# Piece sizes of q and k in the first stage, and the place of ScalarE's two table loads in tile 4

## The chip, the cores and the metric

The kernel runs on one core of a Trainium2 chip. The time is the device time of one execution in microseconds; where several runs are given, it is their median. TensorE multiplies, ScalarE and VectorE work elementwise and move results out of PSUM, GpSimd (POOL) and SyncE (SP) mostly issue DMAs. Each engine works through its own instructions in order and waits on semaphores.

## The reference

Two batches of an attention over channels, whose output goes token by token through a two-layer network:

```python
def _attn_ref(q, k, v, tau):            # each (2, 6016, 256), float32
    qn = q / (np.linalg.norm(q, axis=1, keepdims=True) + 1e-06)
    kn = k / (np.linalg.norm(k, axis=1, keepdims=True) + 1e-06)
    s = kn.transpose(0, 2, 1) @ qn / tau        # 256 x 256 a batch
    s = s - s.max(-1, keepdims=True)
    a = np.exp(s)
    a /= a.sum(-1, keepdims=True) + 1e-09
    return (v @ a).astype(np.float32)

def _moe_ref(x, w_in, w_out, alpha):    # x (12032, 256), w_in (256, 2048), w_out (2048, 256)
    h = x @ w_in
    g = np.maximum(h, 0.0) + alpha * np.minimum(h, 0.0)
    return (g @ w_out).astype(np.float32)
```

## The kernel before

The kernel has two parts. The first, up to about 57 us, reads q and k of batch 0 in 47 blocks of 128 tokens (a block is 128 x 512 numbers, q and k side by side, 256 KB) and makes the scores k^T q with TensorE, a block at a time, into one PSUM bank (`qk_block`, L444). Each of its products is two matmul instructions of float32, so a block is four. The blocks arrive in pieces: `PIECES = [2, 3] + [4] * 10 + [2]` (L51) gives the blocks of each piece, and each piece is one DMA on SP's queue into one of `RING = 7` buffers called `stage` (L279). SP issues the first seven at once; for each later one it waits until TensorE and ScalarE are done with the piece that had the buffer. Behind them on SP's queue stand w_in, v of the first tile and nine `late` blocks of batch 1.

Beside it the norms are made, which need the sums of the squares over the tokens. `SUBS` (L59) cuts every piece in parts of at most two blocks. For each part ScalarE squares it (L775) and VectorE adds the squares to `acc0` (L1053); behind the last, VectorE folds two blocks to one (L1056). TensorE then sums over the partitions with a matrix of ones (`channel_sums`, L473). In TensorE's order the sums stand behind the third piece from the end, that is with two pieces still to go (L570). From the sums go: VectorE's clamp (L934), ScalarE's root (L683) with the load of the exponential's table behind it (L686), VectorE's inverse norms and a diagonal matrix (L941 to L952), TensorE's broadcast of the norms of q (`broadcast_rq`, L479) when all 47 blocks are done, ScalarE's copy of that row (L690), VectorE's scaling of the scores (L960), the exponentials (L695) and TensorE's transposes (`transpose_probs`, L486), which stand behind four late blocks in TensorE's order. In VectorE's order splits and sums of v (L894, L903 to L912) are written between the steps of this chain. Ahead of everything TensorE multiplies zeros (`keep_warm`, L440) and opens the two banks of scores with zeros (L435).

The attention matrix is multiplied into w_in, which gives the matrix M of the network's first layer; products with M are made by a scheme of seven multiplications for a 2 x 2 block product. All operands are split into a high and a low part, and each product is three matmuls (hi hi, hi lo, lo hi).

The second part is the main loop: 12 tiles of up to 1024 tokens, each with 8 groups, G = 0 to 95. A group makes in TensorE's order (L597 to L640) the products in the banks Y, X and Z, then three more into X, each followed or preceded by the second layer's products of the group before (`down`, L538). It takes 45 products of 512 columns. ScalarE copies X out four times a group (`take_x`, L747), once behind each product in X; TensorE's next product in X waits for the copy. Between the copies ScalarE casts the high parts of g (L757) and of v (L659) and, in chosen groups, does other work: in tile 4 (groups 32 to 39) the norms, the root, the exponentials and the transposes of batch 1. Group 33 is `SUMS_G`, in which VectorE makes the sums of the squares; group 34 is `ROOT_G`, in which ScalarE takes the root behind its first copy of X; 35 is `BROADCAST_G`. ScalarE needs a table load ahead of the root and another ahead of the exponentials. Both are brought about by a one-column activation: at the end of group 33 the square root (L859), at the end of group 34 the exponential (L686, `load_exp`).

Of the kernel before, what the change touches and what calls it, by code (L numbers as in the profile page):

```python
# [5 lines left out]
def build(nc, qk, qk_t, v_t, w_in, w_out, small, y_t):  # L6
# [4 lines left out]
    ACT = mybir.ActivationFunctionType  # L11
# [20 lines left out]
    def half_width(T):  # L32
        t = T % TILES
        return HALF if t < TILES - 1 else (N - 2 * HALF * (TILES - 1)) // 2
# [13 lines left out]
    SLOT = {B11: 0, T1: 0, T2: 0, T3: 1, B21: 2, T4: 2, B22: 3}  # L48


    PIECES = [2, 3] + [4] * 10 + [2]  # L51
    assert sum(PIECES) == NBLK
    START = [sum(PIECES[:i]) for i in range(len(PIECES))]
    RING = 7
# [3 lines left out]
    assert LATE + 2 * PAIRS == NBLK  # L58
    SUBS = [(i, n, min(2, PIECES[i] - n)) for i in range(len(PIECES)) for n in range(0, PIECES[i], 2)]  # L59
    PAIR_TILES = (1, 2, 3)  # L60
# [18 lines left out]
    with ctx:  # L79
        def sb(name, shape, dt=fp32):  # L80
            return ctx.enter_context(nc.sbuf_tensor(name, shape, dt))
# [8 lines left out]
        ones = sb("ones", [P, P])  # L90
# [7 lines left out]
        warm = sb("warm", [P, 1])  # L98
# [156 lines left out]
        SUMS_G, ROOT_G, BROADCAST_G, SCALE_G, EXP_G, MOVE_G = (SOFT + n for n in range(6))  # L255
# [14 lines left out]
        def side(k):  # L270
            return sigma_neg if BLOCKS[k][1] else sigma
# [4 lines left out]
        def _(sp):  # L276
            def load_piece(i):
                n0, n1 = START[i], START[i] + PIECES[i]
                sp.dma_start(stage[:, i % RING, 0:PIECES[i], :].rearrange("p n c -> p (n c)"),  # L279
                             qk[0, :, n0 * ROW:n1 * ROW]).then_inc(stage_loaded[i % RING], 16)  # L280
# [57 lines left out]
            sp.dma_start(small_sb[:, :], small[:, :]).then_inc(small_loaded, 16)  # L338
            for i in range(RING, len(PIECES)):
                sp.wait_ge(qk0_summed, i - RING + 1)  # L340
# [305 lines left out]
        def _(act):  # L646
# [34 lines left out]
            def take_root(b):  # L681
                act.wait_ge(sumsq_ready, b + 1)
                nc.scalar.activation(root, sum_sq, ACT.Sqrt).then_inc(root_ready, 1)  # L683

            def load_exp():
                nc.scalar.activation(warm[:, :], ones[:, 0:1], ACT.Exp)  # L686

            def copy_rq(b):
                act.wait_ge(rq_bc_ready, b + 1)
                nc.scalar.copy(rq_row, bc_ps).then_inc(rq_row_ready, 1)  # L690

            def exponentials(b):
                act.wait_ge(max_ready, b + 1)
                for kc in range(CC):
                    nc.scalar.activation(probs[:, kc, :], scores[:, kc, :], ACT.Exp,  # L695
                                         bias=neg_max[:, kc:kc + 1],
                                         accum_out=row_sum[:, kc:kc + 1]).then_inc(exp_ready, 1)
# [39 lines left out]
            def take_x(G, n, k):  # L737
                T, jp = G // JP, G % JP
                H = half_width(T)
                j = 2 * jp + BLOCKS[k][0]  # L740
                act.wait_ge(x_done, 4 * G + n + 1)
                if G > 0:
                    act.wait_ge(g_lo_ready, 4 * (G - 1) + k + 1)
                else:

                    act.wait_ge(sums_ready, 1)
                nc.scalar.mul(h[:, k, 0:H], X[:, 0:H], side(k)[:, j:j + 1]).then_inc(x_copied, 1)  # L747

            def split_g_hi(G, k):
                H = half_width(G // JP)  # L750
                act.wait_ge(g_ready, 4 * G + k + 1)
                if G > 0:
                    act.wait_ge(down_done, 4 * (G - 1) + k + 1)
                else:

                    act.wait_ge(m_done, M_FIRST)
                nc.scalar.copy(g_hi[:, k, 0:H], h[:, k, 0:H]).then_inc(g_hi_ready, 1)  # L757

            def take_y(T, t, oc):
                H = half_width(T)  # L760
                act.wait_ge(down_done, 4 * (JP * T + JP - 1) + 3 + t)
                if T == 0:

                    act.wait_ge(w_lo_ready, FJ)
                else:
                    act.wait_ge(y_stored[t], 16 * T)
                nc.scalar.copy(y_stage[:, t, oc, 0:H], y_ps[t][oc][:, 0:H]).then_inc(y_copied, 1)
# [39 lines left out]
            for G in range(GROUPS):  # L807
                T, jp = G // JP, G % JP
                take_x(G, 0, 0)
                if jp == 1 and T > 0:  # L810
                    take_y(T - 1, 1, 0)
                if G > 0:
                    split_g_hi(G - 1, 3)
                if jp == 1 and T > 0:
                    take_y(T - 1, 1, 1)
                if G == ROOT_G:
                    take_root(1)
                if G == EXP_G:
                    exponentials(1)
                if G == 0:  # L820
                    split_m_hi(0, 1)
                if G == 2:
                    split_m_hi(0, 3)
                if G in M_SPLIT:
                    split_m_hi(*M_SPLIT[G])
                if T + 1 < ALL:
                    for op in (V_ACT_FIRST if T == 0 else V_ACT).get(jp, ()):
                        if T == 0 and op == B11:

                            act.wait_ge(qk1_summed, len(LATE_STEPS))  # L830
                        split_v_hi(T + 1, op)
                take_x(G, 1, 3)
                if G == 0:
                    take_m(0, 2)
                if G in PAIR_AT:
                    split_pair_hi(PAIR_AT[G])
                if G == BROADCAST_G:
                    copy_rq(1)
                if G == MOVE_G:
                    split_at_hi(1)  # L840
                if G in M_AT:
                    take_m(*M_AT[G])
                take_x(G, 2, 1)
                split_g_hi(G, 0)
                if G == 0:
                    split_m_hi(0, 2)
                for n in SQ_AT.get(G, ())[:1]:
                    square_rows(n)
                take_x(G, 3, 2)
                if G == 0:  # L850
                    take_m(0, 3)
                for k in (1, 2) if G < GROUPS - 1 else (2, 1):
                    split_g_hi(G, k)
                if jp == 0 and T > 0:
                    take_y(T - 1, 0, 0)
                for n in SQ_AT.get(G, ())[1:]:
                    square_rows(n)
                if G == SUMS_G:
                    nc.scalar.activation(warm[:, :], ones[:, 0:1], ACT.Sqrt)  # L859
                if G == ROOT_G:  # L860
                    load_exp()
                if G in SLICE_AT:
                    split_slice_hi(SLICE_AT[G])
                for j in W_AT.get(G, ()):
                    split_w_hi(j)
# [331 lines left out]
```

## Time and profile before

| | |
|---|---|
| median of 3 runs | 1076.53 us (1076.34 to 1077.75) |
| the profiled execution, its own time | 1076.63 us |
| its span, first to last instruction | 1074.8 us |
| TensorE matmul, busy | 1070.9 us, 100% |
| TensorE weight load, busy | 906.2 us, 84% |
| VectorE, busy | 847.0 us, 79% |
| ScalarE, busy | 654.6 us, 61% |
| GpSimd, busy | 40.4 us, 4% |

A matmul is counted as busy from its start to its modelled end, and they overlap, so that 100% says that TensorE always has something in hand, not that it never waits. Waits show as idle time of its weight loads (PEld) and as matmuls that take longer than their like. Times in rows are in us from the start of the span; "[0.37 <-ACT ...]" is the idle time of the engine ahead of the instruction, and who ended it.

### The profile page before, as it was taken

The page shows a single profiled execution, that of the slowest core. Times are in us where ns is not written, and L with a number is a line of the kernel's source. Part 1 is how long each engine was busy: PE and PEld are TensorE (multiplying, and loading weights), DVE is VectorE, ACT ScalarE, POOL GpSimd, SP SyncE. Part 2 cuts the span into 40 slices and gives each one's busy share as a digit, 9 for nine tenths or more (in the row PEclk, how much of TensorE's full clock was granted, in tenths as well). Part 3 has the DMA queues.
Part 4 walks back from the last instruction along what each step waited for, and adds up shares of the span by engine and source line. Part 5 has one row for each costly group of instructions (what it writes and reads, how often), then busy time and mean ns, then how long its engine had stood idle before and what let it go on. Part 6 is the DMA issues. An engine that isn't in the chain of part 4 may idle for free.

```text
span 1074.8 us, 13902 instructions
## 1 busy us (share of the span) xinstructions
PE 1070.9 (100%) x4995; PEld 906.2 (84%) x4995; DVE 847.0 (79%) x1349; ACT 654.6 (61%) x1100; POOL 40.4 (4%) x54
## 2 busy tenths in 40 slices
PE   9999999999999999999999999999999999999998
PEld 7888888888888888888998888888888888888898
DVE  6999987877877777787798887777777777787776
ACT  6676677667766555655666655555555555555544
POOL 0000000000000000000000000000000000000000
PEclk9999999999999999999999999999999999999999
DMA  9621154455453102103212101201202202200101
GB/s 382 284 88 50 40 158 127 138 160 150 134 162 99 30 13 54 45 9 79 69 30 73 50 11 49 59 8 52 59 1 59 59 0 54 57 1 10 40 1 35
DMA packets 30837, 80.07 MB, mean 74 GB/s; under 512 B 2992, under 2 KB 9264, under 8 KB 29232
## 3 DMA queue, kind: packets, MB, share of 16 engines
q1 hardware_dynamic: 24288, 67.80, 18.1%
q0 software_dynamic: 6336, 11.28, 6.8%
q8 instruction: 39, 0.64, 0.2%
q14 instruction: 30, 0.25, 0.1%
q10 hardware_dynamic: 144, 0.11, 0.0%
HBM read 64.04 MB, written 12.32 MB: 71 GB/s over the span
## 4 chain that ended last, share of the span: by engine, by line
PE 100%; ACT 0%; issue 0%; POOL 0%; POOLq 0%
PE y_ps L538 47%; PE x_ps L512 24%; PE z_ps L512 12%; PE p_ps L512 6%; PE x_ps L444 4%; PE s_ps L464 3%; PE p_ps L498 2%; PE s_ps L444 1%; PE y_ps L498 1%; PE y_ps L553 0%; PE z_ps L440 0%; PE p_ps L486 0%; PE p_ps L473 0%; PE p_ps L479 0%; ACT y_stage L876 0%; PE s_ps L435 0%
## 5 line engine op out<-in xcount | busy, mean ns | idle before, releaser
L538 PE MATMUL y_ps<-g_hi,w_hi 128*128 128x512 f32 (+1 forms) x760 | 293.1, 386 | 0.0
L538 PE MATMUL y_ps<-g_hi,w_lo 128*128 128x512 f32 (+1 forms) x760 | 292.9, 385 | 0.0
L538 PE MATMUL y_ps<-g_lo,w_hi 128*128 128x512 f32 (+1 forms) x760 | 292.9, 385 | 0.0
L757 ACT CAST g_hi<-h 128x512 fp32r<-128x512 f32 (+1 forms) x384 | 234.0, 610 | 78.6 <-DVE h L1011 69.3
L1011 DVE SCALAR_TENSOR_TENSOR h<-h,small_sb 128x512 f32<-128x512 f32 (+1 forms) x384 | 273.7, 733 | 0.0
L1003 DVE SCALAR_TENSOR_TENSOR h<-z_ps,sigma_neg,h 128x512 f32<-128x512 f32 (+1 forms) x192 | 141.7, 738 | 148.0 <-ACT h L747 147.6
L1045 DVE TENSOR_TENSOR g_lo<-h,g_hi 128x512 fp32r<-128x512 f32 (+1 forms) x384 | 249.9, 670 | 0.8 <-ACT g_hi L757 0.5
L747 ACT ACTIVATE h<-x_ps,sigma_neg 128x512 f32<-128x512 f32 (+1 forms) x192 | 130.7, 681 | 175.2 <-PE x_ps L512 165.1
L747 ACT ACTIVATE h<-x_ps,sigma 128x512 f32<-128x512 f32 (+1 forms) x192 | 130.6, 680 | 124.8 <-PE x_ps L512 120.2
L538 PEld LDWEIGHTS y_ps<-g_hi,w_hi 128*128 128x128 f32 x760 | 142.7, 188 | 27.3 <-issue 0.3
L538 PEld LDWEIGHTS y_ps<-g_hi,w_lo 128*128 128x128 f32 x760 | 142.7, 188 | 27.0
L538 PEld LDWEIGHTS y_ps<-g_lo,w_hi 128*128 128x128 f32 x760 | 142.7, 188 | 26.6
L512 PE MATMUL x_ps<-v_hi,m_hi 128*128 128x512 f32 (+1 forms) x384 | 148.8, 388 | 0.0
L512 PE MATMUL x_ps<-v_lo,m_hi 128*128 128x512 f32 (+1 forms) x384 | 148.1, 386 | 0.0
L512 PE MATMUL x_ps<-v_hi,m_lo 128*128 128x512 f32 (+1 forms) x384 | 148.0, 385 | 0.0
L1003 DVE SCALAR_TENSOR_TENSOR h<-p_ps,sigma,h 128x512 f32<-128x512 f32 (+1 forms) x96 | 70.8, 738 | 42.2 <-ACT h L747 42.2
L512 PEld LDWEIGHTS x_ps<-v_hi,m_hi 128*128 128x128 f32 x384 | 72.1, 188 | 14.4 <-ACT h L747 0.9
L512 PEld LDWEIGHTS x_ps<-v_hi,m_lo 128*128 128x128 f32 x384 | 72.1, 188 | 13.6
L512 PEld LDWEIGHTS x_ps<-v_lo,m_hi 128*128 128x128 f32 x384 | 72.1, 188 | 12.9
L512 PE MATMUL z_ps<-v_hi,m_hi 128*128 128x512 f32 (+1 forms) x192 | 74.3, 387 | 0.0
L512 PE MATMUL z_ps<-v_lo,m_hi 128*128 128x512 f32 (+1 forms) x192 | 74.0, 385 | 0.0
L512 PE MATMUL z_ps<-v_hi,m_lo 128*128 128x512 f32 (+1 forms) x192 | 73.9, 385 | 0.0
(129 smaller groups left out, 1009.4 us busy)
## 6 DMA issues: line engine op xcount, KB each, us to landing
rows_t<-qk_t SPq DMA_DIRECT2D x32, 376.0 KB, 4.0
stage<-qk SPq DMA_DIRECT2D x10, 1024.0 KB, 13.3
v_stage<-v_t SPq DMA_DIRECT2D x20, 512.0 KB, 4.6
y_t<-y_stage SPq DMA_DIRECT2D x20, 512.0 KB, 2.8
pair<-qk SPq DMA_DIRECT2D x19, 512.0 KB, 3.7
v_stage<-v_t POOLq DMA_DIRECT2D x27, 256.0 KB, 4.1
scratch<-w_in SPq DMA_DIRECT2D x12, 256.0 KB, 2.8
v_stage<-v_stage POOLq DMA_DIRECT2D x9, 256.0 KB, 3.3
```

The costliest lines, as they stand in the source:

```text
L444: product = nc.tensor.matmul(s_ps[b][:, kc * C:(kc + 1) * C], rows[:, C + kc * P:C + (kc + 1) * P], rows[:, 0:C], start=False, stop=last, ...
L464: product = nc.tensor.matmul(S[:, kc * C:(kc + 1) * C], k_part[:, i, ks], q_part[:, i, 0:C], start=False, stop=n == PAIRS - 1 and i == 1 a ...
L498: product = nc.tensor.matmul(bank[:, kc * 2 * P:(kc + 1) * 2 * P], a_part[:, qc, kc * P:(kc + 1) * P], w_part[:, qc, :], start=a_part is a ...
L512: product = nc.tensor.matmul(bank[:, 0:H], m_part[:, jp, a, :], v_part[T % 2][:, t, 0:H], start=start and m_part is m_hi and v_part is v_h ...
L538: product = nc.tensor.matmul(y_ps[t][oc][:, 0:H], w_part[:, j, ws], g_part[:, k, 0:H], start=jp == 0 and k < 2 and w_part is w_hi and g_pa ...
L747: nc.scalar.mul(h[:, k, 0:H], X[:, 0:H], side(k)[:, j:j + 1]).then_inc(x_copied, 1)
L757: nc.scalar.copy(g_hi[:, k, 0:H], h[:, k, 0:H]).then_inc(g_hi_ready, 1)
L1003: return nc.vector.scalar_tensor_tensor(out=h[:, k, 0:H], in0=bank[:, 0:H], scalar=side(k)[:, j:j + 1], in1=h[:, k, 0:H], op0=ALU.mult, op ...
L1011: nc.vector.scalar_tensor_tensor(out=h[:, k, 0:H], in0=h[:, k, 0:H], scalar=alpha_sb[:, j:j + 1], in1=h[:, k, 0:H], op0=ALU.mult, op1=ALU. ...
L1045: nc.vector.tensor_tensor(g_lo[:, k, 0:H], h[:, k, 0:H], g_hi[:, k, 0:H].bitcast(fp32), ALU.subtract).then_inc(g_lo_ready, 1)
```

## The change

`PIECES` goes from 2, 3, ten of 4 and 2 to 1, 2, 3, ten of 4 and 1: 14 pieces in place of 13, over the same 47 blocks and the same ring of seven buffers. The loops over the pieces, the parts of at most two blocks (25 in place of 24) and all waits follow from this list. The two activations that bring in the tables in groups 33 and 34 move, in ScalarE's order, from the end of the group to a place behind the second copy of X.

```diff
@@ -48,7 +48,7 @@
-    PIECES = [2, 3] + [4] * 10 + [2]
+    PIECES = [1, 2, 3] + [4] * 10 + [1]
     assert sum(PIECES) == NBLK
@@ -830,6 +830,10 @@
                 take_x(G, 1, 3)
+                if G == SUMS_G:
+                    nc.scalar.activation(warm[:, :], ones[:, 0:1], ACT.Sqrt)
+                if G == ROOT_G:
+                    load_exp()
                 if G == 0:
                     take_m(0, 2)
@@ -855,10 +859,6 @@
                 for n in SQ_AT.get(G, ())[1:]:
                     square_rows(n)
-                if G == SUMS_G:
-                    nc.scalar.activation(warm[:, :], ones[:, 0:1], ACT.Sqrt)
-                if G == ROOT_G:
-                    load_exp()
                 if G in SLICE_AT:
```

## Rows read from the trace of the kernel before

**Rows 1.** The page, chain of work that ended last, shares by engine.
```profile
PE 100%; ACT 0%; issue 0%; POOL 0%; POOLq 0%
```
**Rows 2.** Waits of TensorE's weight loads, 30 us to the end: total, times, longest.
```profile
PEld x_ps L512 <- ACT h L747: 0.9, 3, 0.4
...
PEld p_ps L486 <- ACT scratch L695: 0.4, 1, 0.4
```
**Rows 3.** DMA issues, 0 to 10 us (KB, us to landing); timeline (start, us): first products.
```profile
stage<-qk SPq DMA_DIRECT2D x1, 512.0 KB, 3.8
...
4.62 36.37 PE L444 MATMUL x_ps<-stage 128*128 128x256 f32 x164
```
**Rows 4.** Timeline of TensorE's matmuls in narrow windows, 3 to 10 us.
```profile
3.54 0.63 PE L435 MATMUL x_ps<-zeros 128*128 128x512 bf16 x1
3.96 0.63 PE L435 MATMUL s_ps<-zeros 128*128 128x512 bf16 x1
...
7.81 1.46 PE L444 MATMUL x_ps<-stage 128*128 128x256 f32 x6
```
**Rows 5.** Timeline, 5 to 42 us: SP's reloads, VectorE's sums, fold, low parts.
```profile
7.36 16.73 SPq L279 DMA_DIRECT2D stage<-qk  x6
...
26.20 11.86 DVE L1053 TENSOR_TENSOR acc<-acc,sq 128x1024 f32<-128x1024 f32 x9 [0.28 <-ACT sq L775]
...
38.10 0.69 DVE L1056 TENSOR_TENSOR acc<-acc 128x512 f32<-128x512 f32 x1
...
39.40 2.50 DVE L1024 TENSOR_TENSOR w_raw_lo<-w_raw,w_raw_hi 128x512 fp32r<-128x512 f32 x4
```
**Rows 6.** Timeline, 40 to 51 us: from the channel sums to the transposes.
```profile
40.83 1.05 PE L473 MATMUL p_ps<-ones,acc 128*128 128x128 f32 x8
...
41.92 0.16 DVE L934 TENSOR_SCALAR col<-p_ps 128x4 f32<-128x4 f32 x1
...
46.91 0.59 PE L479 MATMUL p_ps<-scratch,ones 128*128 128x256 f32 x2
46.92 0.69 DVE L909 TENSOR_TENSOR v_stage<-v_stage 128x512 f32<-128x512 f32 x1
...
47.94 0.88 DVE L960 SCALAR_TENSOR_TENSOR scratch<-x_ps,col,scratch 128x256 f32<-128x256 f32 x2 [0.33 <-ACT scratch L690]
...
50.92 0.42 PEld L486 LDWEIGHTS p_ps<-ident,scratch 128*128 128x128 f32 x4 [0.37 <-ACT scratch L695]
```
**Rows 7.** Chain that ended last in order of time, 428 to 470 us.
```profile
438.90 0.68 PE z_ps L512 x3
...
440.94 0.74 PE x_ps L512 x3
...
443.07 0.84 PE x_ps L512 x3
443.91 1.39 PE y_ps L538 x6
```
**Rows 8.** Timeline, 428 to 450 us: ScalarE's copies of X, table loads, VectorE, TensorE.
```profile
428.74 0.69 ACT L747 ACTIVATE h<-x_ps,sigma 128x512 f32<-128x512 f32 x1 [0.17 <-PE x_ps L512]
...
433.50 0.69 ACT L747 ACTIVATE h<-x_ps,sigma_neg 128x512 f32<-128x512 f32 x1 [1.35 <-PE x_ps L512]
...
434.29 0.75 DVE L1003 SCALAR_TENSOR_TENSOR h<-z_ps,sigma_neg,h 128x512 f32<-128x512 f32 x1 [1.94 <-ACT h L747]
...
434.66 0.39 PE L512 MATMUL x_ps<-v_hi,m_hi 128*128 128x512 f32 x1
...
438.58 1.28 ACT L859 ACT_TABLE_LOAD   x1
...
439.99 0.67 ACT L747 ACTIVATE h<-x_ps,sigma 128x512 f32<-128x512 f32 x1
...
442.20 0.69 ACT L747 ACTIVATE h<-x_ps,sigma_neg 128x512 f32<-128x512 f32 x1 [0.48 <-DVE g_lo L1045]
...
448.79 1.28 ACT L686 ACT_TABLE_LOAD   x1
```

## The prediction

> **What bounds the kernel now.** I read the chain of waits on the page first: it ends last through TensorE at 100% of the span [rows 1]. The reader should see there that nothing off TensorE can shorten the kernel; only a stall of TensorE, or work of its own, is worth anything. But this chain also counts a stretched matmul as work, so the second view is the list of what its weight loads waited for, from 30 us on [rows 2]. It holds two small things that touch this diff: three waits on ScalarE's copies of X, 0.9 us together, and one wait of 0.4 us for the exponentials ahead of the transposes. Everything that the change can move lies in three places: the first 7 us, the chain from the channel sums to the transposes (41 to 51 us), and groups 33 and 34 at 428 to 450 us. I take them in that order.
>
> **The start: a first piece of one block.** TensorE's warm-up ends with two matmuls of 512 columns, the openings of the score banks, which start at 3.54 and 3.96 [rows 4]; 512 columns in 0.42 us is the lower of the engine's two levels, 1.2 GHz. (The granted clock of the windows prints 1.00 there too, so I go by the spacing.) The first product of q and k starts at 4.62 [rows 3], as soon as the first piece of two blocks, 512 KB, has landed: 0.74 + 3.8 = 4.54 [rows 3]. One block less is about 0.62 us less of transfer, an estimate from 256 KB at the 426 GB/s that this stretch moves; so it lands near 3.9 and is no longer the limit. The limit is then the opening at 3.96 plus 0.42 = 4.38. TensorE starts 0.24 us earlier.
>
> What is that worth? At the upper level a product's matmuls are 0.216 us apart ((1.46 - 0.38) / 5, [rows 4]). All 164 at that pace would be 163 x 0.216 + 0.38 = 35.6 us; the row says 36.37 [rows 3], so 0.78 us was lost at the start, that is 0.37 on a first step of 0.59 and 0.21 on each of two of 0.43. The clock therefore rose near 4.62 + 0.59 + 2 x 0.43 = 6.07. If it rises at the same time again, TensorE fits between 4.38 and 6.07 about one matmul more: it is ahead by g = 0.2 us from there on. The bounds: 0.14 if the long first step stays, 0.24 if all of it counts; zero if the small piece lands no earlier, since the first packets are slow ones. I take 0.2.
>
> Does TensorE then starve? The pieces stand at 1, 3, 6, 10 and 14 blocks; at 0.62 us each behind 3.9 they land near 5.2, 7.1, 9.6 and 12.1. TensorE (0.864 us a block, four matmuls of 0.216) wants them at 6.1, 7.8, 10.4 and 13.9. No starvation, by 0.6 us at the least. ScalarE squares one more piece and VectorE adds it: the count of instructions goes from 24 to 25, and three of them are of one block instead of one. A sum of two blocks comes every 1.33 us ((11.86 - 1.23) / 8, [rows 5]); for one of one block I estimate 0.8 from half the elements: 22 x 1.33 + 3 x 0.8 against 23 x 1.33 + 0.8 is 0.3 us more. The last fold starts at 38.10 [rows 5] and TensorE comes to the channel sums only at 40.83 [rows 6]; 2 us of cover hide it. VectorE's work behind the fold, the low parts of w_in, ends at 41.90 [rows 5], and would end by 42.2. SP's queue: the reloads of the ring wait for smaller early pieces, but they lie so far ahead of the transfers (issued from 7.36 to 24.1, [rows 5]) that the DMA engines keep a backlog; w_in, v and the late blocks, queued behind, move by 0.1 to 0.4 us at most, and TensorE wants the late blocks only at 47.
>
> **The sums one block later.** This is the part that costs. TensorE takes the channel sums at the third piece from the end. Before, 41 blocks stand ahead of them (2 + 3 + 9 x 4) and 6 behind; now 42 and 5. So the sums start 0.86 - g = 0.66 us later, near 41.49 by [rows 6]. What waits for them: VectorE's clamp at 41.92, which starts just as the sums end, and behind it in VectorE's queue everything up to the end of the mixing at 46.92 + 0.69 = 47.61, a stretch without a gap worth naming; behind ScalarE's root its table load and its copies, which have 3 us to spare. VectorE then stood idle for ScalarE's copy of the norms' row and started the scaling of the scores at 47.94 [rows 6]: 0.33 us, of which 0.04 is handshake. That is all the slack of this chain, 0.3. TensorE's own order (47 blocks, sums, broadcast at 46.91) does not change; it only comes 0.2 earlier. So the scaling starts at max(47.65 + 0.66, 47.94 - 0.2) = 48.3, 0.36 later than before; reduction, exponentials and transposes follow one another without another path, and TensorE's wait ahead of the transposes, 0.37 us at 50.92 [rows 6], starts 0.2 earlier and ends 0.36 later: near 0.93 us. Afterwards every engine stands behind this same point, so the delay is kept. Head: **+0.36 us**, between +0.6 (g = 0, no slack) and -0.2 (the chain has slack I do not see, and g is kept).
>
> **The table loads in tile 4.** The square root's load stands at the end of group 33, ahead of the first copy of X of group 34. It takes 1.28 us at 438.58, and that copy starts at 439.99 [rows 8], where the groups' period of 10.20 (45 matmuls of 0.2267) and the same copy of group 33 [rows 8] put it at 428.74 + 10.20 = 438.94. The delay passes through VectorE's sum and low part to the second copy, at 442.20 instead of 441.66 (431.46 + 10.20, and 431.46 is 433.50 - 1.35 - 0.69), and so into TensorE: in the chain in order of time four pieces of this group are stretched, 0.74, 1.39 (twice) and 0.84, where three matmuls take 0.68 and six 1.36 [rows 7]. That is 0.06 + 0.03 + 0.16 + 0.03 = 0.28 us. The exponential's load at 448.79 [rows 8] stretches nothing: the next group is longer only by its broadcast.
>
> Behind the second copy, ScalarE is idle for 1.35 us before the third, waiting for TensorE [rows 8]. Load and warm-up take 439.99 - 438.58 = 1.41. The third copy is thus late by some 0.06 to 0.1 us in both groups. What is queued behind: that copy, then the casts of g and the fourth copy. TensorE wants the third at 434.66 and it ends at 433.50 + 0.69 = 434.19 [rows 8]; 0.47 us of cover against 0.1. VectorE's add of Z behind it, 434.29 + 0.75, is wanted by the product in Z at 434.66 + 0.68 = 435.34: 0.3 of cover. So the new place costs nothing and the 0.28 comes back. Bounds: 0.15 if the root and the cast keep the second copy late, 0.28 if not. Tile 4: **-0.28 us**.
>
> A rule that speaks against this half: the Trainium skill (ScalarE: Activation LUTs, What ACT_TABLE_LOAD costs) gives each switch 1.28 us for the load and 1.38 for a drain, 2.66 together. The trace agrees on the first and not on the second: the load starts 0.02 behind the end of the cast before it, and the copy follows at once. By the rule the answer would be the last rival below.
>
> **Sum.** 1076.63 us is the profiled execution's own time, its span 1074.8 and 1.8 around it; + 0.36 - 0.28 gives 1076.7. It lies 0.1 above the median of the three runs, so I say **1076.6** for a median. The three runs spread over 1.4 us, more than both terms.
>
> **The rivals.** (a) Forecast, both terms as above: 1076.6, chance 0.50. (b) The first piece brings nothing (its packets are no quicker than the landing seen), and the second copy in group 34 stays half late: + 0.57 - 0.15, 1076.95, slower than before; decided by whether the first product still starts at 4.6. Chance 0.20. (c) The chain behind the sums has more slack than the 0.3, for instance if VectorE's small steps are quicker when nothing else runs: head - 0.2, total - 0.48, 1076.05. Against it speaks the stretch without gaps. Chance 0.12. (d) The clock rises earlier, because TensorE no longer pauses between 4.38 and 4.62; nothing in the trace dates it but the one rise. At most the whole stretch to 6.07 at the upper level: g near 1.0, since each of the four or so slow steps then gives 0.21 more; the sums come earlier than before and everything moves with them: - 0.4 - 0.28, 1075.85. Chance 0.08. The Trainium skill (TensorE: Matmul & The Clock Gate, Part 1) says that the place of the rise varies from run to run; no row here shows that. (e) ScalarE is held for 2.66 us by each load in its new place, from 432.15 to 434.8: the third copy ends 0.95 us after TensorE wants it, in both groups, and the switch decides as soon as it takes over 1.8 us. + 1.9 + 0.36 - 0.28: 1078.5. Chance 0.03. The rest, 0.07, is for what I have not seen, on both sides.
>
> **Range and chances.** 1075.8 to 1077.5 takes in (a) to (d) with their bounds and the spread of a median of three; it leaves out (e) and half the rest. A measurement can tell about 0.2%, 2.15 us, from no change; only (e) and the unseen come near: faster by more than that 0.02, slower 0.03, the same 0.95.
>
> **What would show it.** Right: the first product near 4.4; eight matmuls of the sums near 41.5 and the clamp near 42.6; VectorE no longer idle ahead of the scaling, which starts near 48.3; the wait ahead of the transposes near 0.9 us; the stretched pieces at 441 to 444 back to 0.68 and 1.36; the third copies of groups 33 and 34 less than 0.15 later in their group. Wrong: TensorE waiting for a piece or for the fold, an idle VectorE ahead of the clamp with no later end, a stretched piece around 434 or 445.

## The result and the profile after

The changed kernel takes 1078.28 us in the median of 22 runs (1077.44 to 1079.58), the kernel before, on the same chips, 1077.09 (22 runs, 1076.34 to 1078.03). The ratio is 1.0013, 95% interval 1.0007 to 1.0019: about 1.2 to 1.4 us slower. The forecast was 1076.6, in a range of 1075.8 to 1077.5; it started from a median of 1076.53 for the kernel before, so 0.5 of the 1.7 us between forecast and measurement is that starting value, and the change itself was forecast at about + 0.1 and measured at + 1.2. The profiled execution took 1079.16 us, its span is 1077.3; it lies 0.9 above the median of its kernel, so not all that it shows need belong to the typical run.

The chain of work that ended last is no longer TensorE alone. From the page after:

```profile
PE 98%; DVE 1%; DMA 1%; ACT 0%; issue 0%; SPq 0%; DVEq 0%; ACTq 0%
```

Where [rows 1] had TensorE at 100%, there is now a DMA, and VectorE. The waits of TensorE's weight loads, 5 to 30 us (total, times, longest), where the kernel before has none:

```profile
PEld x_ps L444 <- DMA stage<-qk: 1.4, 1, 1.4
```

The first transfers after (count, KB, us to landing):

```profile
stage<-qk SPq DMA_DIRECT2D x1, 768.0 KB, 7.0
stage<-qk SPq DMA_DIRECT2D x1, 512.0 KB, 3.8
stage<-qk SPq DMA_DIRECT2D x1, 256.0 KB, 2.8
```

The start of the timeline after (start, us, what):

```profile
3.58 0.63 ACT L775 ACTIVATE sq<-stage 128x512 f32<-128x512 f32 x1 [0.48 <-DMA stage<-qk]
...
4.06 1.52 SPq L338 DMA_DIRECT2D small_sb<-small  x1
...
4.39 3.35 PE L444 MATMUL x_ps<-stage 128*128 128x256 f32 x12
...
8.69 1.13 PE L444 MATMUL x_ps<-stage 128*128 128x256 f32 x4 [0.95 <-DMA stage<-qk]
```

The first product starts at 4.39, against 4.62 in [rows 3]: as forecast. But behind three blocks (twelve matmuls) TensorE stands still from 7.7 to 8.7, until the third piece lands; the forecast had it at 7.1. ScalarE waits for the same piece, and VectorE behind it. A stretch by stretch view of both kernels shows why (window, then busy us of five engines with their counts; last three: granted clock, DMA share, GB/s). Before, then after:

```profile
4.00:5.00 1.00, 0.97 (x3) 0.38 (x2) 0.00 (x0) 0.40 (x1) 0.00 (x0) 1.00 1.05 440
5.00:6.00 1.00, 1.00 (x3) 0.80 (x3) 0.23 (x1) 0.66 (x1) 0.00 (x0) 1.00 1.01 424
6.00:7.00 1.00, 1.00 (x6) 0.83 (x5) 0.99 (x1) 0.51 (x1) 0.00 (x0) 1.00 1.06 451
7.00:8.00 1.00, 1.00 (x6) 0.90 (x5) 0.42 (x1) 1.00 (x2) 0.00 (x0) 1.00 0.99 418
```
```profile
4.00:5.00 1.00, 1.00 (x4) 0.82 (x3) 0.68 (x1) 0.22 (x2) 0.00 (x0) 1.00 1.01 385
5.00:6.00 1.00, 1.00 (x5) 0.83 (x4) 0.01 (x1) 1.00 (x1) 0.00 (x0) 1.00 0.88 352
6.00:7.00 1.00, 1.00 (x7) 0.87 (x6) 0.92 (x1) 0.04 (x1) 0.00 (x0) 1.00 1.09 371
7.00:8.00 1.00, 0.73 (x4) 0.30 (x2) 0.30 (x1) 0.00 (x0) 0.00 (x0) 1.00 0.96 344
```

The DMA engines are nearly as busy as before (shares of 0.88 to 1.09 against 0.99 to 1.06) and move 344 to 385 GB/s in place of 418 to 451. By the packets in the traces, nine of the 311 that start between 3 and 8 us take two to five times as long as is usual for their size; before, none of 333 does.

The other places. The channel sums and what follows (after, beside [rows 6]):

```profile
43.55 0.16 DVE L934 TENSOR_SCALAR col<-p_ps 128x4 f32<-128x4 f32 x1 [0.20 <-PE p_ps L473]
...
49.17 0.87 DVE L960 SCALAR_TENSOR_TENSOR scratch<-x_ps,col,scratch 128x256 f32<-128x256 f32 x2
...
52.14 0.42 PEld L486 LDWEIGHTS p_ps<-ident,scratch 128*128 128x128 f32 x4 [0.82 <-ACT scratch L695]
```

VectorE is no longer idle ahead of the scaling, and the wait ahead of the transposes is 0.82 us where it was 0.37. Tile 4, the chain in order of time after (beside [rows 7]):

```profile
442.21 0.68 PE x_ps L512 x3
442.89 1.36 PE y_ps L538 x6
444.25 0.68 PE x_ps L512 x3
```

And the timeline of ScalarE in group 33 after (beside [rows 8]):

```profile
433.41 1.28 ACT L834 ACT_TABLE_LOAD   x1
434.70 0.20 ACT L834 ACTIVATE warm<-ones 128x1 f32<-128x1 f32 x1
434.81 0.67 ACT L747 ACTIVATE h<-x_ps,sigma_neg 128x512 f32<-128x512 f32 x1
```

The stretched pieces are back at 0.68 and 1.36: group 34 takes 10.22 us in place of 10.48. And one place that the forecast did not look at, in tile 5 (batch 1's first M, 549 us). The chain in order of time after:

```profile
547.80 0.35 issue
...
549.18 0.02 DVEq L1128
549.20 0.40 issue
549.60 0.70 DVE h L1003
550.29 0.04 issue
550.34 0.86 PE z_ps L512 x3
```

Before, at the same work, the chain is TensorE without a break:

```profile
548.35 0.62 PE x_ps L512 x3
548.97 0.63 PE z_ps L512 x3
```

Between VectorE's wait, which is over at 549.20, and its add of Z at 549.60 nothing happens for 0.40 us, "issue" in the page's words; before, the same add started 0.05 behind its wait. The product in Z waits for this add. From one fourth copy of X to the next, group 45 takes 11.02 us in place of 10.63.

So the profiled execution reads: + 1.22 us up to the end of group 0 (67.55 against 66.32, the fourth copy of X), - 0.26 in group 34, + 0.39 in group 45, + 0.12 in group 44, and + 0.67 in the last four groups, whose matmuls are 0.2066 apart in place of 0.2027. This last term comes and goes: near the end of the span, e1 has it in four groups, e9 and e10 in three, e13 in two, e2, e8 and e15 in one, most of the others in none. I count it as a matter of the single execution; that is a judgement, not shown.

### The profile page after: what moved, and what is told of

The parts are those of the page before. It is cut to its first block, busy times and chain, and to the rows that moved or that the text cites. A ratio compares the mean times of both kernels' runs of the same rounds, so it can differ in the third digit from the quotient of the medians.

```text
span 1077.3 us, 13908 instructions
## 1 busy us (share of the span) xinstructions
PE 1071.9 (99%) x4995; PEld 906.7 (84%) x4995; DVE 847.2 (79%) x1350; ACT 655.2 (61%) x1101; POOL 40.5 (4%) x54
## 4 chain that ended last, share of the span: by engine, by line
PE 98%; DVE 1%; DMA 1%; ACT 0%; issue 0%; SPq 0%; DVEq 0%; ACTq 0%
PE y_ps L538 47%; PE x_ps L512 24%; PE z_ps L512 12%; PE p_ps L512 6%; PE x_ps L444 3%; PE s_ps L464 3%; PE p_ps L498 2%; DMA stage<-qk 1%; PE y_ps L498 1%; PE y_ps L553 0%; PE s_ps L444 0%; DVE v_lo L894 0%; ACT scratch L695 0%; PE p_ps L486 0%; PE p_ps L473 0%
## 5 line engine op out<-in xcount | busy, mean ns | idle before, releaser
L1003 DVE SCALAR_TENSOR_TENSOR h<-p_ps,sigma,h 128x512 f32<-128x512 f32 (+1 forms) x96 | 70.8, 738 | 41.5 <-ACT h L747 41.4
```

What stands on the lines that cost most here:

```text
L1003: return nc.vector.scalar_tensor_tensor(out=h[:, k, 0:H], in0=bank[:, 0:H], scalar=side(k)[:, j:j + 1], in1=h[:, k, 0:H], op0=ALU.mult, op ...
```

## The experiments

Three questions: does each half cost what was forecast; why does the third piece land late; where does VectorE's pause come from. The table has one row for each kernel, from its own profile: first product, VectorE's clamp, fourth copy of X of group 0 (all us from the start of the span), length of groups 34 and 45, and its ratio to the kernel before where it ran six times or more, or else the time of its one run (the kernel before, on the same chips, took 1076.85 beside e5 and e6, 1077.06 beside e11 and 1077.20, one run, beside e13 to e16).

| kernel | first product | clamp | group 0 | group 34 | group 45 | ratio (95%) |
|---|---|---|---|---|---|---|
| before | 4.62 | 41.92 | 66.32 | 10.48 | 10.63 | |
| after | 4.39 | 43.55 | 67.55 | 10.22 | 11.02 | 1.0013 (1.0007 to 1.0019) |
| e1 pieces 1, 2, 3 ... 1 alone | 4.39 | 43.18 | 67.17 | 10.47 | 11.02 | 1.0012 (1.0003 to 1.0021) |
| e2 loads alone | 4.88 | 41.88 | 66.03 | 10.23 | 10.75 | 0.9997 (0.9988 to 1.0006) |
| e3 pieces 1, 1, 3 ... 2 | 4.39 | 44.78 | 68.78 | 10.49 | 11.02 | 1.0031 (1.0020 to 1.0043) |
| e4 pieces 2, 4 ... 1 | 4.62 | 42.83 | 66.84 | 10.49 | 10.63 | 1.0006 (0.9997 to 1.0015) |
| e5 first piece in two DMAs | 4.40 | 44.44 | 68.59 | 10.47 | 10.63 | one run, 1078.84 us |
| e6 first piece in two halves of rows | 5.56 | 43.76 | 67.74 | 10.47 | 10.63 | one run, 1077.99 us |
| e7 pieces 1, 4 ... 2 | 4.39 | 42.03 | 66.44 | 10.46 | 10.68 | 1.0002 (0.9993 to 1.0011) |
| e8 VectorE shifted | 4.72 | 41.73 | 65.86 | 10.46 | 10.68 | 1.0006 (0.9997 to 1.0015) |
| e9 VectorE shifted, two waits | 4.57 | 41.68 | 66.07 | 10.46 | 10.68 | 1.0005 (0.9996 to 1.0014) |
| e10 after, burst of six | 4.39 | 42.87 | 66.85 | 10.22 | 10.99 | 1.0009 (1.0000 to 1.0018) |
| e11 long burst of issues | 4.43 | 50.04 | 74.01 | 10.47 | 10.75 | one run, 1084.50 us |
| e12 loads, early broadcast | 4.64 | 42.28 | 66.27 | 10.23 | 10.72 | 0.9996 (0.9987 to 1.0005) |
| e13 pieces 4, 1, 1 ... 1 | 5.83 | 44.88 | 68.89 | 10.47 | 10.99 | one run, 1079.86 us |
| e14 pieces 1, 3 ... 3 | 4.39 | 42.33 | 66.32 | 10.47 | 10.99 | one run, 1076.97 us |
| e15 pieces 2, 2, 3 | 4.75 | 41.94 | 66.38 | 10.47 | 10.63 | one run, 1076.88 us |
| e16 third piece held | 4.39 | 42.94 | 66.92 | 10.47 | 10.99 | one run, 1077.80 us |

A warning on the first three columns. TensorE's clock rises at another moment in each profile (6.09 in before, 5.58 in after, 4.55 in e1 and e2, 3.65 to 6.67 in all but e13, by the granted clock and by the spacing of the matmuls, 0.427 us ahead of the rise and 0.216 behind it), and a rise that comes 1 us earlier gives back about 0.5 us. So differences of some tenths in group 0 between two profiles are read with the place of the rise beside them.

### The halves and the two terms of the sum

e1 takes the new list without the moved loads, e2 the moved loads without the new list.

> The new piece list alone, the table loads where they were before. Theory A (the third piece of q and k lands late whenever the first pieces are this small: TensorE waits 1.1 us for it at 8.5 us, as in the profile of after, and the sums come one block later): 1.2 to 1.5 us slower than the kernel before, with a wait of TensorE for a piece near 7.4 us in the trace. Theory B (that wait was a chance of the one profiled execution; only the later sums cost): 0.3 to 0.5 us slower, no such wait.

> The moved table loads alone, pieces as before. If the change of place gives back the stretched matmuls of group 34 and nothing else moves: 0.25 us faster than before, group 34 at 10.20 to 10.23 us in place of 10.48. Rival (it disturbs something later, as the longer groups 44 and 45 in the profile of after): 0 to 0.6 us slower.

e1 is as slow as both together, and TensorE waits for the third piece again (its weight loads 1.0 us, in after 1.4): theory A. But the wait is not the whole of its price. In e1 the clock rose 1.5 us earlier than before, so that TensorE had made up for the wait when it came to block 41; still the clamp is 1.26 us later than before, and it starts 0.55 us behind the sums' end, because VectorE is not done (timelines of VectorE and TensorE in e1):

```profile
40.77 2.50 DVE L1024 TENSOR_TENSOR w_raw_lo<-w_raw,w_raw_hi 128x512 fp32r<-128x512 f32 x4
41.58 1.05 PE L473 MATMUL p_ps<-ones,acc 128*128 128x128 f32 x8
43.18 0.16 DVE L934 TENSOR_SCALAR col<-p_ps 128x4 f32<-128x4 f32 x1
```

The low parts of w_in start 1.37 us later than in [rows 5]. VectorE's own chain of sums stands behind the late piece too and has one part more. In after TensorE ends this wait (sums to 43.51, low parts to 43.35), in e3, e5, e6, e10 and e16 VectorE does, as in e1.

e2 shows the forecast gain in its place, 10.23 us for group 34, but its time is not told from that of the kernel before: the 0.25 us is less than its 11 runs can tell.

```diff
e3: -    PIECES = [2, 3] + [4] * 10 + [2]
    +    PIECES = [1, 1, 3] + [4] * 10 + [2]
e4: +    PIECES = [2, 4] + [4] * 10 + [1]
e7: +    PIECES = [1, 4] + [4] * 10 + [2]
```

> Pieces 1, 1, 3, ten of 4 and 2: the first piece small, the sums at the same block as before (41 ahead, 6 behind), loads as before. Theory A (small first pieces make a later piece land late): 0.5 to 1.2 us slower, with a wait of TensorE for a piece before 10 us. Theory B (a small first piece lets TensorE start 0.24 us earlier and costs nothing): 0.15 to 0.2 us faster, first product near 4.3.

> Pieces 2, 4, ten of 4 and 1: the first piece as before, the sums one block later (42 ahead, 5 behind), loads as before. By the prediction's sum for g = 0: 0.5 to 0.6 us slower, the wait ahead of the transposes near 0.9 us in place of 0.37, the scaling idle-free. Rival (the chain has slack): no slower than 0.1.

> Pieces 1, 4, ten of 4 and 2: a small first piece, then large ones; sums at the same block, as many parts as before (24). Theory D: packets slow at 3 to 7 us, piece 4 lands after 8.5 us, over 1 us slower than before. Theory C or none: TensorE waits some 0.4 us for the second piece (five blocks at 6.4), 0.2 us slower than before at most.

e4 isolates the later sums: from its waits,

```profile
PEld p_ps L486 <- ACT scratch L695: 0.8, 1, 0.8
```

with group 0 ending 0.52 us later and 0.65 us in time (not clear of zero by its interval). The forecast's sum for g = 0 was 0.57. This term was right in place and about right in size: two smaller things nearly cancel in e4's profile, a short wait for its larger second piece (two steps of 0.41 and 0.32 us in place of 0.22) and a clock that rose 0.5 us earlier. e3 keeps the sums where they were and is the slowest of those timed more than once: 3.3 us by the ratio. (Four of its six runs, 1080.6 to 1081.2 us, have a mean granted clock of 0.998; the two at 1.0 took 1078.9 and 1079.7, so 2.1 to 3.0 us of it stand without that.) e7, with the same small first piece but a large second one, is at most 1.2 us slower by its interval and has only a short wait for its second piece:

```profile
PEld x_ps L444 <- DMA stage<-qk: 0.5, 1, 0.5
```

So a small first piece alone does not bring the long wait. What the earlier start is worth, e7 does not show: its first product is 0.23 us earlier, but its sixth matmul starts at 6.62 in place of 6.52, since its clock rose at 6.51 in place of 6.09 (0.2 us) and it waited 0.1 us for the second piece. Three profiles with the first pieces of the kernel before do show what a lead is worth. Their clock rose earlier, their sums start earlier than the 40.83 of [rows 6], and group 0 ends earlier by the same amount: e2 0.31 and 0.29 us, e8 0.46 and 0.46, e9 0.26 and 0.25.

### Why the third piece is late

```diff
 e5, first piece of the kernel before in two DMAs, both awaited:
+                if i == 0:
+                    for part in range(2):
+                        sp.dma_start(stage[:, 0, part, :], qk[0, :, part * ROW:(part + 1) * ROW]
+                                     ).then_inc(stage_loaded[0], 16)
+                    return
 ...
 e6, the same, but 64 partitions and both blocks in each:
+                        ps = slice(part * P // 2, (part + 1) * P // 2)
 ...
```

> The kernel before, but its first piece of two blocks comes as two DMAs of one block each, and TensorE and ScalarE wait for both as for one. Theory D (small rows at the head of the queue make the DMA engines themselves slow, whoever uses the data): packets behind them slow between 3 and 7 us, below 180 KB in each half microsecond in place of 210, a wait of TensorE for the third piece near 7 us, as in the kernel with pieces 1, 1, 3. Theory C (the engines that start early on the small piece disturb the transfers): transfers and first waits as in the kernel before.

> The kernel before, but its first piece comes as two DMAs of 64 partitions each, rows of 4 KB as before. If it is the size of the rows (2 KB against 4 KB) that makes the engines slow: as the kernel before. If it is one more DMA in the queue, or a DMA of half the bytes: slow as the split by blocks.

e5 does what the kernel before does, only its first 512 KB come as two DMAs, and they land 0.2 us sooner. It moves 313 to 379 GB/s from 4 to 8 us (windows of e5), and TensorE waits 3 us for the next piece (waits of e5):

```profile
4.00:5.00 1.00, 1.00 (x4) 0.51 (x3) 0.00 (x0) 0.62 (x1) 0.00 (x0) 1.00 0.81 313
...
7.00:8.00 1.00, 0.00 (x0) 0.00 (x0) 0.00 (x0) 0.00 (x0) 0.00 (x0) 1.00 0.99 358
```
```profile
PEld x_ps L449 <- DMA stage<-qk: 3.7, 2, 3.0
```

Already from 3 to 4 us, when no engine uses q and k yet, it moves 344 GB/s against 426 before. The engines that use the data are thus not the cause. e6 is slow too, though not as long (166, 350, 391 and 410 GB/s; its waits for pieces: 2.7 us), with rows of 4 KB as before: the size of the rows is not needed for it. Its halves of 64 partitions may do something of their own, so it carries less weight.

The next two ask whether it is SP's issuing beside the transfers (its eighth issue took 1.52 us after, 0.45 before).

```diff
 e10, on the changed kernel:
             for i in range(RING):
+                if i == 6:
+                    sp.wait_ge(stage_loaded[2], 16)
                 load_piece(i)
 e11, on the kernel before:
             sp.dma_start(small_sb[:, :], small[:, :]).then_inc(small_loaded, 16)
+            for part in range(len(LATE_PARTS)):
+                load_late(part)
+            load_v(0)
 ... (and their calls further down go)
```

> The changed kernel, but SP issues six pieces at once and holds the seventh and what is behind it until the third has landed; the DMA engines keep work until 14 us. Theory B (the transfers are slow when the third DMA of the queue moves while SP still issues its first ones): now SP is done at 3.4 us, ahead of the third piece at 3.9; packets at full pace, third piece lands near 7.1, no wait of TensorE for it, first part 1.1 us shorter than in the changed kernel, time 0.2 to 0.5 us above the kernel before. Rival (small DMAs are slow by themselves): slow as the changed kernel, 1.2 us above the kernel before.

> The pieces of the kernel before, but v of the first tile and the late blocks are issued right behind the small constants, so that SP issues twelve DMAs without a wait, until about 6.5 us. Theory B: the third piece starts to move at 5.4 us, while SP still issues: packets slow from then on, issues of 1 us and more, third piece of four blocks lands after 9.6 in place of 9.0. Rival: packets at full pace to the end. The total time says nothing here, since the late blocks now stand ahead of the eighth piece and TensorE waits for it later.

Both went against theory B. In e10 SP is silent from 3.6 us until the third piece has landed, and the transfers are slow all the same (330, 332, 352, 367 GB/s in the four windows from 4 to 8 us); its time, 0.85 us above the kernel before by the medians, lies between the two expectations. In e11 SP issues without a pause to 6.9 us, and they run at full pace:

```profile
5.00:6.00 1.00, 1.00 (x6) 0.87 (x5) 0.42 (x1) 0.47 (x1) 0.00 (x0) 1.00 1.06 442
```

(e11's time of 1084.5 us says nothing of this: its weight loads wait 4.5 us for a later piece, and behind that wait the granted clock is at the lower level, 0.50, from 29.0 to 35.8 us.) The long issue is a companion of the slowness, not its cause. The last four vary the sizes and the time alone.

```diff
e13: +    PIECES = [4, 1, 1] + [4] * 10 + [1]
e14: +    PIECES = [1, 3] + [4] * 10 + [3]
e15: +    PIECES = [2, 2, 3] + [4] * 10
e16: the new list, and
             for i in range(RING):
+                if i == 2:
+                    sp.wait_ge(stage_loaded[0], 16)
                 load_piece(i)
```

> Pieces 4, 1, 1, ten of 4 and 1. Theory E (slow when the third DMA of the queue starts to move within some 3 us of the first packet): here the third starts near 5.0 us; packets at full pace, about 210 KB in each half microsecond from 3 us on. Theory S (two DMAs of at most two blocks one behind the other): slow, 160 to 180 KB in each half microsecond from 5 us on. The time says little, TensorE starts 1.2 us later.

> Pieces 1, 3, ten of 4 and 3: one small DMA, then one of three blocks; the third starts near 4.8 us. Theory S: full pace, as pieces 1, 4. Theory E: at its border, full pace or a little slow. Sums one block earlier in the order than before.

> Pieces 2, 2, 3 and ten of 4: no piece of one block, two of two; the third starts near 4.3 us. Both theories say slow: 160 to 190 KB in each half microsecond between 4 and 7 us, third piece (seven blocks) later than 7.7 us. If it is at full pace, the border lies between 3.9 and 4.3 us, or at the piece of one block.

> The new piece list, loads as before, but SP issues the third piece only when the first has landed (near 3.9 us), so that its packets start near 5. Theory E: full pace from 5 us on, third piece lands near 7.3 although the engines paused half a microsecond. Theory S: slow packets as in the changed kernel, third piece at 8.3 or later.

e14 and e15 run at full pace (434 and 436 GB/s from 7 to 8 us), e15 against both expectations. e13 has 346 GB/s from 5 to 6 us, while its two pieces of one block pass, and 457 in the next: small DMAs behind a large one do no lasting harm. e16 lies between its two expectations. It is slow from 4 to 6 us, where theory E wanted full pace from 5, then at full pace with the very list that is slow otherwise, and its third piece lands at 7.64 (expected near 7.3 by E, 8.3 or later by S):

```profile
4.00:5.00 1.00, 1.00 (x5) 0.86 (x4) 0.69 (x1) 0.37 (x2) 0.00 (x0) 1.00 0.96 199
5.00:6.00 1.00, 1.00 (x7) 0.87 (x6) 0.16 (x1) 0.81 (x1) 0.00 (x0) 1.00 0.75 270
6.00:7.00 1.00, 1.00 (x6) 0.70 (x4) 1.00 (x1) 0.00 (x0) 0.00 (x0) 1.00 1.08 449
```

That leans to theory E. The rule that fits the profiles was read off them after the runs, and no run was made to try it: the six kernels whose first two DMAs hold three blocks or fewer (768 KB: after, e1, e3, e5, e6, e10) are slow up to 6 or 8 us, and the ten with four or more (before, e2, e4, e7, e8, e9, e11, e12, e14, e15) are not; e13 and e16 are the two just told. By the packets in the traces, the third DMA begins at 3.4 to 4.3 us in the slow ones, at 4.45 in e16 and at 4.6 or later in the others. Size and time go together in all but e16, so which of them counts is not shown. What happens inside the queue or the engines the trace does not say either, and this stays open.

How a rate that is lower by a sixth makes a piece 1.5 us late, the packets do say. Their size tells the piece (a row of one block is 2 KB, of two 4, of three 6, of four 8). In the kernels at full pace a piece lands 0.3 to 0.8 us behind the moment at which the DMA engines have moved as many bytes in all (before: 5.79 and 6.47, 8.24 and 8.97). In after the bytes of six blocks are moved at 6.68, so in step the third piece would have landed near 7.0 to 7.5 (an estimate), about as forecast and ahead of TensorE's need at 7.7. It landed at 8.64: packets of the fourth piece run from 5.90 on, beside those of the third, whose last one ends at 8.30, and 656 KB of the fourth have been begun by then. e3 lands 2.3 us behind its bytes and e5 3.1; in e1, e6 and e10 it is 0.8 to 0.95, and there most of the delay is the rate. A piece is in only when its last packet is, and here the engines did not stay in step.

### VectorE's pause

```diff
e8:              dve.wait_ge(const_ready, 3)
+                dve.wait_ge(zeros_ready, 2)
+                nc.vector.tensor_copy(row_max, ones[:, 0:CC])
e9: the same with one more wait, on ident_zeroed
```

> The kernel before with one more wait and one two-column copy at the head of VectorE's program, which shifts the places of all its later instructions by what the new piece list shifts them. Theory: group 45 becomes 0.39 us longer (11.02 in place of 10.63), with 0.35 us between VectorE's wait and its add at 548 us, as in all three kernels with 25 parts; nothing else changes; 0.3 to 0.4 us slower. Rival: these 0.39 us come from something else of the new pieces; then group 45 stays at 10.63.

> The kernel before with two more waits and one two-column copy at the head of VectorE's program: a shift by two of its records, as in the changed kernel, where the last one was by one and moved the pauses to groups 52 and 88. Theory (a pause of 0.35 us stands at fixed places of VectorE's program): the pause at 548 us, group 45 at 11.02 us in place of 10.63, and another pause near 711 us without effect. Rival: group 45 stays at 10.63 to 10.7.

The place was missed, twice; the thing was not. With one more instruction at the head of VectorE's program group 45 stays at 10.68, but pauses of the same kind appear at 286, 622 and 990 us, and the one at 622 stretches group 52 from 10.23 to 10.55 us. The chain there in e8, with three matmuls into Z that take 0.68 in the kernel before:

```profile
623.93 0.95 PE z_ps L512 x3
```

Group 88 grows by 0.24 in the same way. e9's second wait left no instruction of its own in the trace (1588 of VectorE's records as in e8, 1587 before, 1589 after), so it repeated e8's shift by one record and did not give the shift by two that it was made for. Counted in these records from 0, the waits ahead of the pauses stand at 830 and 1086 in the changed kernel and at 446, 958 and 1470 in e8 and e9, all whole multiples of 128 apart. And group 45 splits the kernels without exception: 10.99 to 11.02 us in the seven whose list makes 25 parts (after, e1, e3, e10, e13, e14, e16), 10.63 to 10.75 in all with 24. The rule holds in all 18 profiles: of the records 62, 190, 318 and so on, every 128th, those that are a wait have the pause of 0.40 us behind them, 20 of 20, and no other wait has one of 0.385 to 0.405 us. In the nine kernels with 24 parts and no shift none of these records is a wait, and none has the pause. (Other idle times behind finished waits, of 0.25 to 0.6 us, stand at much the same instructions before and after.) And the trace holds what comes with it: 8 KB packets of the queue whose kind it calls "instruction". One of them starts 0.66 to 0.92 us behind the start of the delayed instruction in all 20 cases (550.26 and 712.69 in the changed kernel). The kernel before has such packets near the same records (549.08 at record 830), but there VectorE runs its instructions back to back. That reads as a fetch of VectorE's instructions, 128 at a time, which a stretch of work hides and a wait does not. It is argued from this coincidence: no run moved the packet without the pause.

### A version that might beat both

```diff
e12, the kernel before with the moved loads, and
                 for n in range(count):
+                    if START[i] + n == NBLK - 1:
+                        broadcast_rq(0)
 ...
-            broadcast_rq(0)
```

> The kernel before with the moved table loads, and with TensorE's broadcast of the norms ahead of the last block of q and k in place of behind it. If the chain behind the sums is as read (VectorE free at 47.61, slack 0.33): the scaling starts 0.3 us earlier, the wait ahead of the transposes goes from 0.35 to below 0.1, group 34 at 10.22; together 0.5 us faster than before. Rival (the broadcast waits for the diagonal, or the scaling is bound by VectorE at the old time): 0.25 us faster or less.

e12 is 0.5 us faster by its medians (1076.58 against 1077.06), but the interval reaches to 1.0005, and its trace does not show the gain in the first part: group 0 ends at 66.27. Its rows of VectorE say why:

```profile
39.87 2.49 DVE L1025 TENSOR_TENSOR w_raw_lo<-w_raw,w_raw_hi 128x512 fp32r<-128x512 f32 x4
42.28 0.15 DVE L935 TENSOR_SCALAR col<-p_ps 128x4 f32<-128x4 f32 x1
```

TensorE's sums ended at 41.5 here (they start at 40.46), and VectorE came to the clamp only at 42.28, behind the low parts of w_in. In the kernel before both were ready within 0.02 us of each other. The broadcast moved, but VectorE's own chain then ends the wait.

## Why the prediction was wrong

- **"Does TensorE then starve? ... No starvation, by 0.6 us at the least."** This is the step that failed. It carried the pace of [rows 3], 0.62 us a block, over to another list of DMAs. The third piece landed at 8.64 in place of 7.1. The wait that follows is 1.1 us of matmul time in the changed kernel, and e1 and e10 have it too at 0.7 and 0.9 us. The forecast named it as what would show it wrong, and priced it at nothing. The pace itself was lower (344 to 385 GB/s against 418 to 451), and the forecast let a piece land in step with the bytes moved, while in after the packets of the fourth piece ran beside those of the third.
- **"2 us of cover hide it", and the low parts that "would end by 42.2".** The same late piece went through VectorE: its low parts end at 43.35 in after and at 43.27 in e1. e14, with 25 parts and no late piece, has them at 42.41, near the forecast; the rest is the piece.
- **A term that was missing.** "The count of instructions goes from 24 to 25" was weighed for its 0.3 us of VectorE's time only. The part more, two of VectorE's records, shifts all that stand behind it, and a wait that the product in Z hangs on came to stand at a record with a pause, 0.40 us in place of 0.05: + 0.39 us in group 45 (e14 and e15, alike in group 0 within 0.06, have 10.99 and 10.63).
- **The sums one block later:** right in place and about right in size. e4's profile gives + 0.52 for g = 0, forecast 0.57; the wait ahead of the transposes is 0.82, forecast 0.93.
- **The earlier start, g = 0.2:** the first product at 4.39, forecast 4.38; in the changed kernel the lead is gone in the wait for the third piece, so its worth was not measured there. Where TensorE leads by its clock and nothing else changes, the lead is kept (e2, e8 and e9 above), as the forecast took it. Its limit is VectorE, which in the kernel before ends its work on w_in just when the sums end: in e12 TensorE starts the sums 0.37 us earlier, finds VectorE busy, and group 0 ends only 0.05 earlier.
- **The table loads, - 0.28:** - 0.26 in the trace of after and - 0.25 in e2. The third copy of group 33 is late by 0.07 in its group (434.81 - 429.98, against 433.50 - 428.74), as forecast. The drain of 1.38 us that the Trainium skill states (ScalarE: Activation LUTs, What ACT_TABLE_LOAD costs) does not appear at the new place either: the load starts 0.02 behind the copy.
- **The sum put together again:** 0.85 to 1.2 for the first part (e1 and after), 0.39 for group 45, - 0.26 for group 34: 1.0 to 1.35 us. Measured: 1.2 by the medians, 1.4 by the ratio. Of the first part 0.5 is the later sums (e4) and 0.3 to 0.7 the late piece. The second share swings with the clock's rise and is not cleanly priced: e10, with the late piece and an early rise, ends group 0 where e4 does (66.85 and 66.84).
- **The rivals:** (b), 1076.95, and (e), 1078.5, forecast a slower kernel. (e) comes nearest by number, by luck, since its drain of 1.38 us is not there; (b) gets the direction, but the first product does start at 4.39 and group 34 gets its full 0.26 back. What (d) rests on, a clock that rises earlier, did happen (5.58 in after, 4.55 in e1), and the late piece hid it. No rival had a late piece.

## What to carry to other kernels

A transfer rate read in one list of DMAs holds for that list; where the first DMAs of a program change in size, the landing of the later ones is an unknown; here they came 0.7 us (e1) to 2.8 us (e5, against the same piece before) late. A piece has landed only when its last packet has, so bytes divided by rate is the earliest time and not the likely one. No finer split of the head was shown to be faster here (e14 and e15, one run each, lie 0.2 and 0.3 us below the one run beside them, which is within the spread); those with 1 MB or more in the first two DMAs left the transfers at full pace, but for one window of e13. And before an earlier start of one engine is credited, ask which other engine's work meets it at the next joint: here VectorE was level with TensorE to 0.02 us.

## What the runs showed of the hardware

- With 768 KB or less in the first two DMAs of SP's queue, the core's DMA engines moved 289 to 385 GB/s in the windows from 4 to 8 us (e6, with its halves, 166 to 410; e16, with its pause, 199 to 449), with 1 MB or more 393 to 455 (e13 346 in one window); after 6 us the DMA share is about the same in both (0.86 to 1.12 against 0.97 to 1.06). This rests on one profile of each kernel, 18 in all. Splitting one DMA of 512 KB in two, with nothing else changed, made TensorE wait 3.0 us. The engines can run out of step: 656 KB of the fourth piece were begun before the last packet of the third had ended (after).
- Pauses of 0.40 us (0.35 more than usual) between a finished wait and the next instruction of VectorE stand wherever a wait falls on certain records, 128 apart, 20 times in 18 profiles, each with an 8 KB packet of the "instruction" kind 0.66 to 0.92 us behind the delayed instruction's start; one instruction more at its head moved them, and made two groups 0.57 us longer together (e8's profile; its ratio of 1.0006 is not told from 1).
- The spacing of the first products shows the clock rising to the upper level between 3.7 and 6.7 us in the profiles of kernels that begin alike (3.9 in e8, 6.1 in the kernel before, 6.5 in e7), and at 9.1 in e13, where TensorE stood idle from 4.4 to 5.8; each microsecond of delay is half a microsecond of matmul work (0.427 against 0.216 us a step). That is up to 1.5 us, more than either term of the forecast, and may be part of the 1.7 us over which the runs of one kernel spread; the runs without a profile do not show it.
